# Chunk rows loaded in four pieces from ScalarE, and two VectorE steps moved, in a fused attention, MLP and soft-expert kernel

## The chip, the cores and the metric

The kernel runs on one core of one Trainium2 chip. The metric is the device time of one execution in microseconds, lower is better. Three runs of the kernel before took 622.63, 623.71 and 618.45 us (median 622.63). Device time is a little longer than the span of the profile, which goes from the first to the last instruction.

## The reference

Three stages in a row, all in float32. The first is a recurrence over 768 steps for each of 4 x 8 heads of width 48; the other two are an MLP of width 2048 on 3072 tokens of width 384, and soft experts with 32 slots.

```python
for t in range(S):                                   # attention, S = 768
    kt, vt, rt, wt = (k[:, :, t], v[:, :, t], r[:, :, t], w[:, :, t])
    cur = np.einsum('bhd,bhe->bhde', u[None] * kt, vt)
    y[:, :, t] = np.einsum('bhd,bhde->bhe', rt, state + cur)
    state = wt[:, :, :, None] * state + np.einsum('bhd,bhe->bhde', kt, vt)
...
h = x @ w_in                                         # MLP, x = y as 3072 x 384
x = (h * (1.0 / (1.0 + np.exp(-1.702 * h)))) @ w_out
...
logits = x @ phi                                     # soft experts
d = softmax(logits, over tokens);  c = softmax(logits, over slots)
slot_out = relu((d.T @ x) @ w1[e]) @ w2[e]           # for each expert's slots
out = c @ slot_out
```

## The kernel before

**Tiling.** The sequence of each batch is cut in 6 chunks of 128 steps, 24 chunks in all. For each chunk the four arrays w, r, k, v lie in one tile `raw[n % 2]` of 112 partitions (two heads of 48, with a gap) by 4 fields by 4 head pairs by 129 numbers, 903 KB; there are two such tiles. VectorE makes from it the running products of the decays (`decays`, a scan), their inverses (`invert`, a scan), r times decay (`decayed`), k times inverse (`grown_keys`), the bonus products r*u*k (`bonus`), and v times their sum over a head (`bonus_values`, tile `ybuf`). TensorE turns the keys (`turn_keys`), sums the bonus products, and in `meet(o, n)` does the scores and state sums of chunk n together with the outputs of chunk o. Then VectorE adds the outputs to `ybuf`, SyncE stores them to a scratch array and loads them back as columns x of the MLP.

**The MLP.** The chunks are grouped in 9 steps of 2, 2, 2, 3, 3, 3, 3, 3, 3 chunks (256 or 384 columns). Each step has 16 blocks (`NF`), one for every 128 of the 2048 hidden units, so there are 144 blocks, numbered F. In block F TensorE does the first layer of F (9 matmuls: `hps`, line 1377) and the second layer of F - 2 (6 or 9 matmuls: `acc`, line 1512). ScalarE does the activation `g` (line 845) and its rounded part `gh` (line 856), VectorE the rest `gl` (line 1149). Matmuls use split values (a high and a low part), so each product is three matmuls.

**Order.** There is no scheduler. A table written by hand, `part_at`, says in which block F each step of each chunk is issued (`place_parts`), and `meeting_at` says in which block the meetings lie. Within a block each engine goes through its own list of `if` statements in the order written. With f = 16 i the first block of step i, the meetings lie in blocks f + 3, f + 7 and f + 11, and the `bonus` steps one block ahead of each, in f + 2, f + 6 and f + 10.

**Who waits for whom.** The eighth bank of PSUM, `mps`, is used in turn by many steps; `mps_read` is what TensorE waits for before it writes there again. After the bonus sums it is `uv_done`, which `bonus_values` counts (line 1017). So a meeting waits on TensorE until `bonus_values` of the block before is done. `uv_done` is also what SyncE waits for before it loads a chunk's rows (`load_raw`, line 633) into the tile that the chunk two before has left. SyncE's queue holds, one after the other, those loads, the stores of `ybuf` (line 645), the loads of `vn` (line 640) and those of x (line 649). `rest_x` (line 539) makes the low part `xl` of x, which TensorE waits for at the start of a step.

Of the kernel before, what the change touches and what calls it, by code (L numbers as in the profile page):

```python
# [59 lines left out]
def attention_mlp_soft_experts(nc, dmaj, vnat, wall, ucol, w_in, w_out, phi, w1, w2, scratch, out):  # L60
# [8 lines left out]
    with ctx:  # L69
# [144 lines left out]
        decays_first = sem("decays_first")  # L214
        raw_in = [sem(f"raw_in{i}") for i in range(2)]
        vn_in = [sem(f"vn_in{i}") for i in range(2)]
        u_in = sem("u_in")
# [143 lines left out]
        place_parts(5, scan=17, invert=18, grow=18, turn=20, decayed=19, bonus_a=19, bonus_b=19, split=20, bonus=21)  # L361
        place_parts(6, scan=21, invert=22, grow=22, turn=24, decayed=24, bonus_a=23, bonus_b=23, split=24, bonus=25)
        meeting_at = {5: (None, 2), 9: (2, 3), 10: (3, None), 18: (None, 4), 22: (4, 5), 26: (5, 6)}
        for i in range(2, NST - 1):
            n, f = BASE[i + 1] + 1, NF * i
            place_parts(n, scan=f - 6, invert=f - 5, grow=f - 5, bonus_a=f - 3, bonus_b=f - 2, decayed=f - 1,
                        turn=f, split=f, bonus=f + 2)
            place_parts(n + 1, scan=f + 1, invert=f + 2, grow=f + 3, bonus_a=f + 4, bonus_b=f + 4, decayed=f + 5,
                        turn=f + 5, split=f + 5, bonus=f + 6)
            meeting_at[f + 3], meeting_at[f + 7], meeting_at[f + 11] = (n - 1, n), (n, n + 1), (n + 1, None)  # L370
            if i + 1 < NST - 1:
                place_parts(n + 2, scan=f + 6, invert=f + 7, grow=f + 7, bonus_a=f + 8, bonus_b=f + 8, decayed=f + 9,
                            turn=f + 9, split=f + 9, bonus=f + 10)
                meeting_at[f + 11] = (n + 1, n + 2)
# [256 lines left out]
        def _(sp):  # L631
# [43 lines left out]
            for n in range(NCH):  # L675
                if n <= FULL:
                    sp.wait_ge(uv_done, n + 1)
                    load_raw(n + 2)
                if FULL <= n < NCH - 3:
                    sp.wait_ge(uv_done, n + 2)  # L680
                    load_raw(n + 3)
                sp.wait_ge(y_done, n + 1)
# [87 lines left out]
        def _(act):  # L770
# [17 lines left out]
            def excesses(j):  # L788
# [48 lines left out]
            for F, gather, job in slots_of_work:  # L837
# [29 lines left out]
                if job == "exps":  # L867
                    exp_slots(act, 0)
                elif job not in (None, "shares"):
                    if job == 0:  # L870
                        act.wait_ge(y_stored[1], 32 * (NCH // 2 - 1))
                    high_slots(act, job)
                if (F, "split") in part_at:
                    n = part_at[F, "split"]
# [58 lines left out]
        def _(dve):  # L933
# [8 lines left out]
            def field(n, q):  # L942

                return raw[n % 2][:, q, :, 1:C + 1]

            def decays(n):

                if n == 0:
                    dve.wait_ge(decays_first, 16)
                else:  # L950
                    dve.wait_ge(raw_in[n % 2], 16 * (n // 2 + 1))
                flat = [t.rearrange("d p t -> d (p t)") for t in (decay[n % 2][:, :, :], raw[n % 2][:, W], restart[:, :, :])]
                dve.tensor_tensor_scan(flat[0], flat[1], flat[2], 1.0, ALU.mult, ALU.max).then_inc(scanned, 1)  # L953

            def bonus(n, half):

                if n == FULL and half == 0:
                    dve.wait_ge(u_in, 16)
                dve.wait_ge(raw_in[n % 2], 16 * (n // 2 + 1))
                for p in (2 * half, 2 * half + 1):  # L960
# [18 lines left out]
            def decayed(n):  # L979

                if n == 0:
                    dve.wait_ge(raw_in[0], 16)
                if n >= 2 * PRE:
# [6 lines left out]
            def grown_keys(n):  # L990

                dve.wait_ge(inverted, n + 1)
                dve.tensor_tensor(out=kd[n % 2][:, :, :], in0=field(n, KK), in1=inv[:, :, 1:C + 1], op=ALU.mult).then_inc(front, 1)

# [15 lines left out]
            def bonus_values(n):  # L1010

                dve.wait_ge(u_done, n + 1)
                if n >= 2 * PRE:
                    dve.wait_ge(y_stored[n % 2], 32 * (n // 2 - 1))
# [128 lines left out]
            for F, gather, job in slots_of_work:  # L1143
                if F is not None and F < NF * NST:
                    wide = SIZES[F // NF] * C
                    dve.wait_ge(gh_done, F + 1)
                    if F >= 2:
                        dve.wait_ge(mlp_done, F - 1)
                    dve.tensor_tensor(out=gl[F % 2][:, 0:wide], in0=g32[F % 2][:, 0:wide], in1=gh[F % 2][:, 0:wide].bitcast(fp32),  # L1149
                                      op=ALU.subtract).then_inc(gl_done, 1)  # L1150
                if (F, "scan") in part_at:
                    decays(part_at[F, "scan"])
                if (F, "invert") in part_at:
                    invert(part_at[F, "invert"])
# [18 lines left out]
                if F in low_at:  # L1173
                    low_part(low_at[F])
                if (F, "bonus") in part_at:
                    bonus_values(part_at[F, "bonus"])
                if F in meeting_at:
# [3 lines left out]
                    if n is not None:  # L1181
                        first_state(n)
                        mask_scores(n)
                        next_state(n)
                if F is not None and F < NF * NST and split_now(F):
# [552 lines left out]
```

## Time and profile before

| | us |
|---|---|
| median of 3 runs | 622.63 |
| lowest and highest | 618.45, 623.71 |
| the profiled execution | 620.75 |
| its span | 619.0 |

| Engine | busy us | share of the span |
|---|---|---|
| TensorE matmuls (PE) | 579.4 | 94% |
| TensorE weight loads (PEld) | 529.1 | 85% |
| VectorE (DVE) | 329.7 | 53% |
| ScalarE (ACT) | 261.0 | 42% |
| GpSimd (POOL) | 10.4 | 2% |

The mean granted clock of TensorE over the span is 0.984 of full speed. The DMA engines move 77.5 MB, 125 GB/s on average. A matmul in the profile overlaps the next, so its mean duration (340 ns) is longer than the distance between two (about 170 ns). "issue" as the releaser of a wait means that the profile shows nothing that the engine waited for. Issuing a DMA is not counted as busy time of the engine that does it.

### The profile page before, as it was taken

The numbers are of one execution on the slowest core, as the hardware profiler recorded it, in microseconds if no ns is written. First come the engines' busy times: TensorE is split into PE (matmuls) and PEld (weight loads), VectorE is DVE, ScalarE is ACT, GpSimd is POOL, SyncE is SP. The second block draws the span as 40 slices with busy tenths as digits, with TensorE's granted clock in tenths as the row PEclk, the third lists the DMA queues.
The fourth block names the chain that finished last, engine by engine and source line by source line (L and its number), as shares of the span: only waits on it lengthen the run. The fifth ranks groups of instructions, "written<-read, shape, count | busy, mean of one in ns | idle before, by whom it ended". The sixth has DMA issues, their size and how long they took to land.

```text
span 619.0 us, 15142 instructions
## 1 busy us (share of the span) xinstructions
PE 579.4 (94%) x6335; PEld 529.1 (85%) x6335; DVE 329.7 (53%) x713; ACT 261.0 (42%) x540; POOL 10.4 (2%) x28
## 2 busy tenths in 40 slices
PE   8989899799799999998999999997999999999993
PEld 6888888789689998998999999997999999998432
DVE  8688766557565664555545663665344323323314
ACT  4864443263343335333453335332533356554313
POOL 4010000000000000000000000000000000000000
PEclk9999999899899999999999999998999999999998
DMA  8995524304232331033303330333001089668637
GB/s 300 364 247 147 154 61 105 95 2 134 65 100 70 92 95 43 28 83 89 101 1 99 100 100 2 100 99 99 1 3 40 26 296 338 207 204 268 225 121 305
DMA packets 45301, 77.50 MB, mean 125 GB/s; under 512 B 3296, under 2 KB 32480, under 8 KB 42656
## 3 DMA queue, kind: packets, MB, share of 16 engines
q1 hardware_dynamic: 44432, 73.37, 38.2%
q0 software_dynamic: 800, 3.15, 1.5%
q8 instruction: 51, 0.84, 0.6%
q14 instruction: 18, 0.15, 0.1%
HBM read 67.46 MB, written 9.04 MB: 124 GB/s over the span
## 4 chain that ended last, share of the span: by engine, by line
PE 79%; DMA 9%; issue 5%; DVE 3%; ACT 2%; SPq 2%; ACTq 0%; DVEq 0%
PE hps L1377 31%; PE acc L1512 30%; DMA spare<-w_in 3%; DMA w2s<-w 2%; PE mps L1318 2%; DMA y_scratch<-ybuf 2%; PE zps L1300 2%; PE mps L1411 1%; PE mps L1595 1%; PE zps L1312 1%; PE mps L1628 1%; PE yps L1312 1%; DMA out<-obuf 1%; PE mps L1608 1%; PE hps L1672 1%
## 5 line engine op out<-in xcount | busy, mean ns | idle before, releaser
L1149 DVE TENSOR_TENSOR gl<-g,gh 128x384 fp32r<-128x384 f32 (+1 forms) x144 | 73.8, 513 | 228.5 <-ACT gh L856 228.3
L1377 PE MATMUL hps<-xh,wi_hi 128*128 128x384 f32 (+1 forms) x432 | 147.7, 342 | 3.7 <-DVE xl L539 2.0
L1377 PE MATMUL hps<-xh,wi_lo 128*128 128x384 f32 (+1 forms) x432 | 138.3, 320 | 9.3 <-issue 9.3
L1377 PE MATMUL hps<-xl,wi_hi 128*128 128x384 f32 (+1 forms) x432 | 137.9, 319 | 0.0
L845 ACT ACTIVATE g<-hps 128x384 f32<-128x384 f32 (+1 forms) x144 | 65.5, 455 | 168.0 <-PE hps L1377 167.7
L1512 PE MATMUL acc<-wo_hi,gh 128*128 128x384 f32 x384 | 130.3, 339 | 1.1 <-issue 1.1
L1512 PE MATMUL acc<-wo_hi,gl 128*128 128x384 f32 x384 | 130.6, 340 | 0.0
L1512 PE MATMUL acc<-wo_lo,gh 128*128 128x384 f32 x384 | 130.6, 340 | 0.0
L856 ACT ACTIVATE gh<-g 128x384 fp32r<-128x384 f32 (+1 forms) x144 | 70.5, 489 | 122.8 <-PE acc L1512 122.2
L1377 PEld LDWEIGHTS hps<-xh,wi_hi 128*128 128x128 f32 x432 | 82.1, 190 | 17.3 <-issue 8.9
L1377 PEld LDWEIGHTS hps<-xh,wi_lo 128*128 128x128 f32 x432 | 82.0, 190 | 3.5 <-issue 3.5
L1377 PEld LDWEIGHTS hps<-xl,wi_hi 128*128 128x128 f32 x432 | 82.3, 191 | 0.9
L1512 PEld LDWEIGHTS acc<-wo_hi,gh 128*128 128x128 f32 x384 | 73.2, 191 | 2.8 <-issue 2.7
L1512 PEld LDWEIGHTS acc<-wo_lo,gh 128*128 128x128 f32 x384 | 73.2, 191 | 1.3 <-issue 1.2
L1512 PEld LDWEIGHTS acc<-wo_hi,gl 128*128 128x128 f32 x384 | 73.2, 191 | 0.0
L977 DVE TENSOR_TENSOR_SCAN inv<-raw,ends 112x516 f32<-112x516 f32 x24 | 29.6, 1233 | 0.8
L953 DVE TENSOR_TENSOR_SCAN decay<-raw,restart 112x516 f32<-112x516 f32 x24 | 29.4, 1225 | 0.1
L1318 PE MATMUL mps<-vn,kn 64*48 64x48 f32 x640 | 24.0, 206 | 4.1 <-issue 4.0
L1318 PEld LDWEIGHTS mps<-vn,kn 64*48 64x48 f32 x640 | 20.6, 121 | 4.5 <-issue 4.1
L961 DVE SCALAR_TENSOR_TENSOR ruk<-raw,ucols 112x128 f32<-112x128 f32 x80 | 23.2, 345 | 0.0
L1312 PE MATMUL zps<-rp,state 48*48 48x64 f32 x320 | 21.8, 216 | 0.0
L1300 PEld LDWEIGHTS zps<-rp,kd 48*64 48x64 f32 x352 | 12.5, 134 | 9.8 <-issue 9.8
(251 smaller groups left out, 742.8 us busy)
## 6 DMA issues: line engine op xcount, KB each, us to landing
raw<-dmaj SPq DMA_DIRECT2D x23, 903.0 KB, 5.6
w1s<-w SPq DMA_DIRECT2D x16, 768.0 KB, 6.5
w2s<-w SPq DMA_DIRECT2D x16, 768.0 KB, 6.9
vn<-vnat SPq DMA_DIRECT2D x24, 192.0 KB, 3.2
tests<-wall SPq DMA_DIRECT2D x6, 768.0 KB, 14.9
out<-obuf SPq DMA_DIRECT2D x12, 384.0 KB, 3.9
y_scratch<-ybuf SPq DMA_DIRECT2D x44, 96.0 KB, 2.2
x<-y_scratch SPq DMA_DIRECT2D x22, 192.0 KB, 2.6
```

Of the source, the lines that this page charges most:

```text
L845: act.activation(g32[F % 2][:, 0:wide], hps[F % 2][:, 0:wide], ACT.Gelu_apprx_sigmoid).then_inc(gelu_done, 1)
L856: act.activation(gh[F % 2][:, 0:wide], g32[F % 2][:, 0:wide], ACT.Copy).then_inc(gh_done, 1)
L953: dve.tensor_tensor_scan(flat[0], flat[1], flat[2], 1.0, ALU.mult, ALU.max).then_inc(scanned, 1)
L961: last = dve.scalar_tensor_tensor(ruk[n % 2][:, p, :], field(n, RR)[:, p], ucols[:, p:p + 1], field(n, KK)[:, p], ALU.mult, ALU.mult)
L977: dve.tensor_tensor_scan(flat[0][:, ::-1], later, flat[1][:, ::-1], 1.0, ALU.mult, ALU.add).then_inc(inverted, 1)
L1149: dve.tensor_tensor(out=gl[F % 2][:, 0:wide], in0=g32[F % 2][:, 0:wide], in1=gh[F % 2][:, 0:wide].bitcast(fp32), op=ALU.subtract).then_inc ...
L1300: return pe.matmul(score_banks(n)[par][cols, p * HALF:(p + 1) * HALF], kd[n % 2][rows, p, cols], rp[n % 2][rows, p, cols], start=p == 0, s ...
L1312: return pe.matmul((zps, yps)[c][rows, p * HALF:(p + 1) * HALF], (state[o % 2], midway)[c][rows, p, :], rp[o % 2][rows, p, HALF * c:HALF * ...
L1318: return pe.matmul(sum_banks(n)[c][HALF * par:HALF * par + D, p * D:(p + 1) * D], kn[n % 2][rows, p, HALF * par:HALF * par + D], vn[n % 2] ...
L1377: last = pe.matmul(hps[F % 2][:, 0:wide], w[:, g, at:at + 128], v[i % 2][:, g, 0:wide], start=m == 0, stop=m == 3 * G - 1)
L1411: last = pe.transpose(mps[:, p * R:(p + 1) * R], kd[n % 2][:, p, :], ident[0:R, 0:R])
L1512: last = pe.matmul(acc[m][:, 0:DM], a[k][:, rows], w[:, f % CW, :], start=f == 0 and w is hi and a is gh, stop=f == NF - 1 and a is gl)
```

## The change

Three parts.

1. From chunk 4 on, a chunk's rows are no longer loaded by one DMA of 903 KB from SyncE, but by four of 226 KB from ScalarE, one for each field, in four different blocks given by `load_w`, `load_k`, `load_r`, `load_v` in the table. Each waits for the last reader of its field two chunks before, and each has its own semaphore (`field_in`), for which VectorE waits ahead of each use of the field. Bytes and destinations are the same. Chunks 0 to 3 are loaded as before. SyncE's waits for `uv_done` at those places go with the loads.
2. On VectorE, `bonus_values` stands directly behind `gl` of its block, ahead of the scans and the other steps of that block.
3. For chunk 2 (`PRE`), the mask of the scores and the next state are made in block 7, behind the keys of chunk 3, instead of in block 5.

```diff
+        field_in = [[sem(f"{name}_in{i}") for i in range(2)] for name in ("w", "r", "k", "v")]
...
+        place_parts(PRE, mask=7)
+        place_parts(4, load_w=7, load_k=8, load_r=9, load_v=10)
+        place_parts(5, load_w=15, load_k=16, load_r=17, load_v=18)
+        place_parts(6, load_w=19, load_k=20, load_r=21, load_v=23)
...
             place_parts(n, scan=f - 6, invert=f - 5, grow=f - 5, bonus_a=f - 3, bonus_b=f - 2, decayed=f - 1,
-                        turn=f, split=f, bonus=f + 2)
+                        turn=f, split=f, bonus=f + 2, load_w=f - 8, load_k=f - 7, load_r=f - 6, load_v=f - 4)
             place_parts(n + 1, scan=f + 1, invert=f + 2, grow=f + 3, bonus_a=f + 4, bonus_b=f + 4, decayed=f + 5,
-                        turn=f + 5, split=f + 5, bonus=f + 6)
+                        turn=f + 5, split=f + 5, bonus=f + 6, load_w=f - 2, load_k=f - 1, load_r=f, load_v=f + 1)
...
                 place_parts(n + 2, scan=f + 6, invert=f + 7, grow=f + 7, bonus_a=f + 8, bonus_b=f + 8, decayed=f + 9,
-                            turn=f + 9, split=f + 9, bonus=f + 10)
+                            turn=f + 9, split=f + 9, bonus=f + 10, load_w=f + 2, load_k=f + 4, load_r=f + 5, load_v=f + 6)
...
             for n in range(NCH):
-                if n <= FULL:
+                if n < PRE:
                     sp.wait_ge(uv_done, n + 1)
                     load_raw(n + 2)
-                if FULL <= n < NCH - 3:
-                    sp.wait_ge(uv_done, n + 2)
-                    load_raw(n + 3)
                 sp.wait_ge(y_done, n + 1)
...
+            def load_field(n, q):
+
+                wide = HP * (C + 1)
+                part = slice(q * wide + (q == RR), (q + 1) * wide + (q == W))
+                dst, src = (t.rearrange("d q p t -> d (q p t)") for t in (raw[n % 2], dmaj[n]))
+                act.dma_start(dst[:, part], src[:, part]).then_inc(field_in[q][n % 2], 16)
...
+                if (F, "load_v") in part_at:
+                    n = part_at[F, "load_v"]
+                    act.wait_ge(uv_done, n - 1)
+                    load_field(n, VV)
...
+                if (F, "bonus") in part_at:
+                    bonus_values(part_at[F, "bonus"])
                 if (F, "scan") in part_at:
                     decays(part_at[F, "scan"])
...
                 if (F, "grow") in part_at:
                     grown_keys(part_at[F, "grow"])
+                if (F, "mask") in part_at:
+                    mask_scores(part_at[F, "mask"])
+                    next_state(part_at[F, "mask"])
...
-                if (F, "bonus") in part_at:
-                    bonus_values(part_at[F, "bonus"])
```

What the diff doesn't tell is where the rows land on each engine. VectorE in block 17, where chunk 4's `bonus_values` (`ybuf<-mps,raw`, whose end TensorE's meeting in block 18 waits for) and chunk 5's first scan (`decay<-raw,restart`) both lie. Before:

```order
L1149 TENSOR_TENSOR gl_115<-g_1_110,gh_112 128x256
L953 SCALAR_TENSOR_TENSOR decay_71<-raw_67,restart 112x516
L1017 TENSOR_TENSOR ybuf_87<-mps,raw_68 112x512
L1149 TENSOR_TENSOR gl_114<-g_0_109,gh_111 128x256
L973 RECIPROCAL ends<-decay_71 112x4
L977 SCALAR_TENSOR_TENSOR inv<-raw_67,ends 112x516
```

The same place in the changed kernel:

```order
L1185 TENSOR_TENSOR gl_115<-g_1_110,gh_112 128x256
L1053 TENSOR_TENSOR ybuf_87<-mps,raw_68 112x512
L987 SCALAR_TENSOR_TENSOR decay_71<-raw_67,restart 112x516
L1185 TENSOR_TENSOR gl_114<-g_0_109,gh_111 128x256
L1008 RECIPROCAL ends<-decay_71 112x4
L1012 SCALAR_TENSOR_TENSOR inv<-raw_67,ends 112x516
```

The scan now stands behind `ybuf`. In the blocks f + 2 it is `RECIPROCAL` and the scan `inv` that stood ahead of `ybuf` and now stand behind it.

SyncE's queue around chunks 2 and 3, where the store of chunk 3's outputs (`y_scratch<-ybuf_87`) stands behind a load of rows. Before:

```order
L649 DMA x<-y_scratch 128x3x128
L633 DMA raw_68<-dmaj 112x2064 [waits uv_done]
L645 DMA y_scratch<-ybuf_87 48x4x128 [waits y_done]
L645 DMA y_scratch<-ybuf_87 48x4x128
L649 ISA [waits y_stored1]
```

The same place in the changed kernel:

```order
L654 DMA x<-y_scratch 128x3x128
L650 DMA y_scratch<-ybuf_87 48x4x128 [waits y_done]
L650 DMA y_scratch<-ybuf_87 48x4x128
L654 ISA [waits y_stored1]
```

The load is gone from this queue, and with it its wait. ScalarE in blocks 15 to 18, where the four loads of chunk 5 now lie (in the kernel before there was no DMA among these rows):

```order
L865 ACTIVATE gh_112<-g_1_110 128x256 [waits mlp_done,gelu_done]
L802 DMA raw_68<-dmaj 112x517 [waits inverted]
L854 ACTIVATE g_0_109<-hps 128x256 [waits gl_done,h_done]
L865 ACTIVATE gh_111<-g_0_109 128x256 [waits mlp_done,gelu_done]
L802 DMA raw_68<-dmaj 112x516 [waits ruk_made,front]
L904 ACTIVATE rukh<-ruk_79 112x512 [waits u_done,ruk_made]
L811 ACTIVATE kn_83<-mps 128x448 [waits meetings,kd_turned]
L854 ACTIVATE g_1_110<-hps 128x256 [waits gl_done,h_done]
L861 ACTIVATE x_116<-acc 128x384 [waits mlp_done]
L861 ACTIVATE x_116<-acc 128x384
L865 ACTIVATE gh_112<-g_1_110 128x256 [waits mlp_done,gelu_done]
L802 DMA raw_68<-dmaj 112x515 [waits ruk_made,decayed_done]
```

Each load stands directly behind `gh` of its block, ahead of the block's other steps. TensorE's instructions are the same ones in the same order.

## Rows read from the trace of the kernel before

**Rows 1.** The page's first lines, and the queue that fetches instructions: packets, MB, share.
```profile
span 619.0 us, 15142 instructions
PE 579.4 (94%) x6335; PEld 529.1 (85%) x6335; DVE 329.7 (53%) x713; ACT 261.0 (42%) x540; POOL 10.4 (2%) x28
...
q8 instruction: 51, 0.84, 0.6%
```

**Rows 2.** Waits of the matmuls, all that matter here: us in total, times, longest.
```profile
PE hps L1377 <- issue: 9.3, 3, 3.4
PE mps L1318 <- issue: 4.0, 1, 4.0
PE zps L1300 <- DVE ybuf L1017: 2.7, 4, 0.9
PE hps L1377 <- DVE xl L539: 2.0, 1, 2.0
...
PE mps L1411 <- DVE kd L993: 1.1, 1, 1.1
...
PE zps L1300 <- issue: 1.1, 1, 1.1
PE acc L1512 <- issue: 1.1, 1, 1.1
```

**Rows 3.** Windows, four idle stretches: length, busy us of each engine, PEclk, DMA share, GB/s.
```profile
109.96:113.92 3.96, 0.05 (x2) 0.05 (x4) 0.07 (x1) 0.00 (x0) 0.00 (x0) 1.00 0.32 90
155.58:158.89 3.31, 0.05 (x1) 0.06 (x1) 1.50 (x5) 0.00 (x0) 0.00 (x0) 1.00 0.51 115
281.38:283.96 2.58, 0.06 (x1) 0.06 (x1) 1.52 (x5) 0.00 (x0) 0.00 (x0) 1.00 0.38 83
426.52:429.94 3.42, 0.05 (x1) 0.04 (x1) 2.58 (x8) 0.00 (x0) 0.00 (x0) 0.82 0.46 116
```

**Rows 4.** Timeline of SyncE's queue: start, duration; three of five loads of rows.
```profile
106.91 0.33 SPq L633 DMA_DIRECT2D raw<-dmaj  x1
...
276.74 0.33 SPq L633 DMA_DIRECT2D raw<-dmaj  x1
...
422.94 0.33 SPq L633 DMA_DIRECT2D raw<-dmaj  x1
```

**Rows 5.** DMA view of 419 to 427.3 us: busy tenths in 40 slices, then the queues.
```profile
DMA  0000000000000000000000092093798999595967
...
q1 hardware_dynamic: 118, 0.92, 39.1%
```

**Rows 6.** DMA view of the next 1.7 us, 427.3 to 429.
```profile
q8 instruction: 1, 0.02, 4.8%
```

**Rows 7.** Windows at half clock, and one of the same length behind the first.
```profile
114.76:118.18 3.42, 3.42 (x15) 3.42 (x15) 2.48 (x8) 0.38 (x1) 0.00 (x0) 0.51 0.38 85
118.18:121.60 3.42, 3.42 (x27) 3.42 (x26) 2.71 (x5) 1.34 (x4) 0.00 (x0) 1.00 0.29 93
...
429.94:435.62 5.68, 5.68 (x20) 5.58 (x20) 0.00 (x0) 0.84 (x2) 0.00 (x0) 0.50 0.27 76
```

**Rows 8.** Timeline of VectorE in block 17.
```profile
81.66 1.23 DVE L953 TENSOR_TENSOR_SCAN decay<-raw,restart 112x516 f32<-112x516 f32 x1
82.80 0.67 DVE L1017 TENSOR_TENSOR ybuf<-mps,raw 112x512 f32<-112x512 f32 x1
```

**Rows 9.** The chain that ended last: start, us; chunk 3's store.
```profile
65.62 5.75 DMA y_scratch<-ybuf
```

**Rows 10.** Timeline of VectorE where step 1 of the MLP begins.
```profile
74.60 0.56 DVE L539 TENSOR_TENSOR xl<-x,xh 128x384 fp32r<-128x384 f32 x1 [0.92 <-ACT xh L447]
```

**Rows 11.** The page's last part: count, KB, median us to landing.
```profile
y_scratch<-ybuf SPq DMA_DIRECT2D x44, 96.0 KB, 2.2
...
raw<-dmaj SPq DMA_DIRECT2D x1, 226.2 KB, 2.7
```

**Rows 12.** A group of ScalarE: busy us, mean ns, idle us before it and releaser.
```profile
L856 ACT ACTIVATE gh<-g 128x384 fp32r<-128x384 f32 (+1 forms) x144 | 70.5, 489 | 122.8 <-PE acc L1512 122.2
```

More of the change, by code:

```diff
@@ L872, in _ @@
                     high_slots(act, job)
+                if (F, "load_w") in part_at:
+                    n = part_at[F, "load_w"]
+                    act.wait_ge(inverted, n - 1)
+                    load_field(n, W)
+                if (F, "load_k") in part_at:
+                    n = part_at[F, "load_k"]
+                    act.wait_ge(front, n - 1)
+                    act.wait_ge(ruk_made, n - 1)
+                    load_field(n, KK)
+                if (F, "load_r") in part_at:
+                    n = part_at[F, "load_r"]
+                    act.wait_ge(decayed_done, n - 1)
+                    act.wait_ge(ruk_made, n - 1)
+                    load_field(n, RR)
+                if (F, "load_v") in part_at:
+                    n = part_at[F, "load_v"]
+                    act.wait_ge(uv_done, n - 1)
+                    load_field(n, VV)
                 if (F, "split") in part_at:
@@ L944, in field, with await_field @@
                 return raw[n % 2][:, q, :, 1:C + 1]
+            def await_field(n, q):
+                if n < FULL:
+                    dve.wait_ge(raw_in[n % 2], 16 * (n // 2 + 1))
+                else:
+                    dve.wait_ge(field_in[q][n % 2], 16 * (n // 2 - FULL // 2 + 1))
             def decays(n):
@@ L950, in decays @@
                 else:
-                    dve.wait_ge(raw_in[n % 2], 16 * (n // 2 + 1))
+                    await_field(n, W)
                 flat = [t.rearrange("d p t -> d (p t)") for t in (decay[n % 2][:, :, :], raw[n % 2][:, W], restart[:, :, :])]
@@ L958, in bonus @@
                     dve.wait_ge(u_in, 16)
-                dve.wait_ge(raw_in[n % 2], 16 * (n // 2 + 1))
+                await_field(n, RR)
+                await_field(n, KK)
                 for p in (2 * half, 2 * half + 1):
@@ L979, in decayed @@
             def decayed(n):
-                if n == 0:
-                    dve.wait_ge(raw_in[0], 16)
+                await_field(n, RR)
                 if n >= 2 * PRE:
@@ L992, in grown_keys @@
                 dve.wait_ge(inverted, n + 1)
+                await_field(n, KK)
                 dve.tensor_tensor(out=kd[n % 2][:, :, :], in0=field(n, KK), in1=inv[:, :, 1:C + 1], op=ALU.mult).then_inc(front, 1)
@@ L1012, in bonus_values @@
                 dve.wait_ge(u_done, n + 1)
+                await_field(n, VV)
                 if n >= 2 * PRE:
@@ L1182, in _ @@
                         first_state(n)
-                        mask_scores(n)
-                        next_state(n)
+                        if n != PRE:
+                            mask_scores(n)
+                            next_state(n)
                 if F is not None and F < NF * NST and split_now(F):
```

## The prediction

> **What bounds the kernel now.** I read the page's head first: matmuls are busy 94% of the span [rows 1], and between about 100 and 560 us the blocks of the MLP follow each other on TensorE without a gap that VectorE or ScalarE causes, save a few. TensorE's own work is not touched by the change. So the question is only which idle stretches of TensorE go, and which come.
>
> The waits of the matmuls [rows 2] give the list. In the MLP region four lines carry it. First, 14.4 us in five stretches with the releaser "issue": 9.3 us in three before `hps`, 4.0 before `mps`, 1.1 before `acc`. Second, 2.7 us in four stretches before a meeting, for `ybuf` of line 1017, and one more stretch of 1.1 us before a meeting (`zps`, "issue"). Third, 2.0 us for `xl` when step 1 begins. Fourth, 1.1 us for `kd`.
>
> The first item is the large one, and its name tells nothing. The windows show the four longest: they begin at 109.96, 155.58, 281.38 and 426.52 us [rows 3], and in them TensorE has nothing to do. SyncE's queue [rows 4] issued a load of a chunk's rows at 106.91, 276.74 and 422.94 us, 3.05, 4.64 and 3.58 us ahead of such a stretch; for the second and for the fifth (1.1 us, in step 3) it is the same, so all five follow a load. The DMA view says what lies between. From 419 to 427.3 us it lists the hardware queue alone, 118 packets, and the engines are full from the load's first packet to the end of that window [rows 5]; no instruction packet. In the next 1.7 us there is one, on q8 [rows 6]. That queue brought 0.84 MB in 51 packets, 16 KB each, and TensorE has 12,670 matmuls and weight loads, about 250 for each packet [rows 1]. My reading: TensorE ran out of instructions, because the block that it had asked for stood behind 903 KB of rows. A meeting, with its many small matmuls back to back, uses them up fastest. And the load falls just there because one event, `uv_done`, starts both the load and the meeting.
>
> The idleness costs twice. Behind the first and the last of the four stretches the granted clock is at its lower level, 1.2 of 2.4 GHz: 3.42 us with 15 matmuls, against 27 in the 3.42 us behind it, and 5.68 us at 0.50 while TensorE is busy throughout [rows 7]; behind the second it is 3.42 us again. The three idle stretches that it follows are those of 3.31, 3.42 and 3.96 us; behind the one of 2.58 us [rows 3] it does not fall.
>
> **The change part by part.**
>
> *Loads in four.* Removed: 20 loads of 903 KB from SyncE. Added: 80 of 226 KB from ScalarE, the same bytes. Three things come of it.
>
> (a) No load is issued by `uv_done` any more. The pieces before a meeting (blocks f + 2, f + 6, f + 10) are issued behind `gh` of their block, about a block ahead of the meeting, and each should keep the DMA engines busy for a quarter of the 3.5 us or so that the whole one fills in [rows 5] (17 of 40 slices of 8.3 us), 0.9 us. The fetch should then start at once. What it needs after that is bounded by rows: at the last long stretch its packet starts after 427.3 and TensorE is back at 429.94, so at most 2.6 us. The time from the old load's issue to the end of the instructions was 3.05, 3.58 and 4.64 us. With 2.6 us nothing is left; if the fetch takes 1 us to start, 3.6 us, the first keeps 0.5 us; with 2 us, 1.5 and 1.0 us. I take 1.0 us left of 14.35 (3.96 + 3.31 + 2.58 + 3.42 + 1.08): **-13.35 us**. Bounds: 14.35 if nothing is left, 8 if pieces, stores and `vn` loads still delay some.
>
> (b) With no stretch of 3.3 us the clock has no reason to fall. At half clock half of the work's time is lost: (3.42 + 3.42 + 5.68) / 2 = **-6.25 us**. Bounds: 6.25, and 0 to 3 if one or two long ones stay.
>
> (c) SyncE's queue is relieved. Chunk 3's store took 5.75 us to land [rows 9], right behind the load of chunk 5, where 2.2 is the median [rows 11]. Up to 3.5 us come off, and x lands that much earlier. But VectorE was idle only 0.92 us for `xh` before `xl` [rows 10]; before that it was in the scan of chunk 4. So of TensorE's 2.0 us, 0.92 go: **-0.95 us** with rounding. Bounds 0 (a piece of chunk 4 beside chunk 2's store) and 2.0. Later steps have x long before.
>
> What it costs: 80 issues at 0.33 us [rows 4] are 27 us on ScalarE, and four waits per chunk. ScalarE sat idle 122.8 us just before `gh` [rows 12] (0.85 us in a block); the issue stands behind `gh`, so `gl` isn't behind it, and what it takes comes out of the wait before the next `gh`. Taken at nothing; should that cover fail, a block loses what an issue exceeds 0.85 us by. The waits name steps at least 3 blocks back, so they find their counts reached. VectorE's new waits: every piece has 2 blocks or more until its first use, 5 to 7 us, and 226 KB landed in 2.7 us at the start of the kernel among others [rows 11]. Nothing.
>
> *Bonus behind `gl`.* In block 17 the scan takes 1.23 us ahead of `ybuf` [rows 8], and TensorE sits idle from 82.66 us until it ends. In the other four stretches a scan stands ahead in the same way. The scans are longer than each of the waits (0.9 at most, and 1.10), so all of 2.7 + 1.1 = **-3.80 us** goes. The sums it reads are done before `gl` is, since TensorE does them right behind the matmuls that `gh` waits for. The scan comes 0.6 us later, with a block to spare. Bounds 2.5 and 3.8. In the blocks of 384 columns nobody waited, but the earlier `uv_done` lets TensorE's queue run on sooner, which is on the side of (a).
>
> *Mask of chunk 2.* About 1 us of VectorE goes from block 5 to block 7. Ahead of `kd` of chunk 3, `gl` of block 7 waits for `gh` anyway, so `kd` comes when it came and the wait of 1.1 us stays; behind it, `decayed` and the products of chunk 3 come 1 us later, still ahead of their meeting. 0; bounds -1.1 and +1.0.
>
> **Sum:** 619.0 - 13.35 - 6.25 - 0.95 - 3.80 = 594.65 us of span. Around it lie 1.75 us (620.75 - 619.0), so 596.4. The profiled execution is 1.9 us under the median of the three; I say **597**.
>
> **A rule that speaks against it.** The Trainium skill, "DMA: Bandwidth & Descriptors", Rules for kernel authors, wants transfers of 1 MiB or more, and says that spreading them over the issuing engines doesn't help bandwidth. By it the change is a step back. No row here makes bandwidth the limit, since the rows are moved a block or more before their use; by the rule the sum would be the same.
>
> **Rivals.**
>
> *The stalls have another cause.* The load and the end of the instructions would both follow from `uv_done`, without one holding up the other. Then stalls and clock stay, and only (c) and the bonus count: 620.75 - 4.75 = 616. For it: one queue's packets needn't stop another's. Against it: in 419 to 427.3 us no instruction packet moved though TensorE ran dry at 426.52, and one came as the load ended [rows 5, 6]. The Trainium skill, "DMA: Bandwidth & Descriptors", Queues, rings and completion order, says that each engine takes turns between queues packet by packet, and "Runtime: NRT & Kernel Launch", Instruction fetch mechanics, that fetches of 16 KiB are mostly hidden; by these this rival is the right one. The size agrees with the 0.84 MB in 51 packets; hidden they were not, by the rows above. Chance 0.11.
>
> *Part of it stays.* One or two long stretches remain, with their fall of the clock, because a piece meets a store and a `vn` load at a fetch: 3.4 + 2.8 us each, so 603 to 609. Chance 0.14.
>
> *More collisions, slower.* A piece has as many rows as the whole had, only shorter ones. If what holds a fetch up is the number of rows queued and not their bytes, a piece blocks as long as a load did, and there are 80 instead of 20. Five of 20 loads hit before. Say the five stay and as many come anew, at (14.35 + 6.25) = 20.6 us for five: 620.75 - 4.75 + 20.6 = 637. It decides from a hold of 3 us for a piece. Against it: 226 KB landed in 2.7 us, issue and all, where 903 KB take twice that. Chance 0.05.
>
> *Forecast*, 592 to 602: chance 0.70.
>
> **Range.** Around 597: all gains at their upper bounds give 594.4 (14.35, 6.25, 3.8 and 2.0 off 620.75), and the executions before scatter by some 2 us around it, so 592. Upwards I go over the case of stalls that stay in part, to 610; outside lie 616, 637 and a little below 592. A measurement of this kernel tells 1%, 6 us, from no change. Faster by more (under 616.4): the forecast, the part case, and half of the first rival, 0.89. Within 1%: the other half, 0.06. Slower: 0.05.
>
> **What would show it.** Right: no wait for "issue" of over 1.5 us among the matmuls between 100 and 560 us; granted clock 1.00 there; no wait of a meeting for `ybuf`; chunk 3's store lands in about 3 us; ScalarE's idle time before `gh` shrinks by less than the 27 us of issues and no line of matmuls waits for `g` or `gl` anew. Wrong: "issue" waits at the same places (then the load was not the cause), instruction packets that still start late beside a piece, DMA issues on ScalarE of over 1 us, or VectorE waiting for `raw`.

## The result: 3.9% faster, and the profile after

Four runs of the changed kernel gave a median of 597.6 us (595.2 to 598.4), beside 622.2 us (618.5 to 623.7) for the kernel before on the same chip. The ratio is 0.961, with a 95% interval from 0.955 to 0.966. The profiled execution took 598.3 us, with a span of 596.6. The forecast was 597. Medians here and below are of all runs on record; the ratios leave out two slow ones, one of experiment 5 and one of the kernel before beside experiments 9 to 11.

The head of the page and the queues come first. TensorE is busy for 96% of the span [rows 1], and `q10` is ScalarE's queue, which is new: 10,240 packets, 128 for each of 80 pieces.

```profile
span 596.6 us, 15329 instructions
PE 573.4 (96%) x6335; PEld 523.4 (88%) x6335; DVE 329.6 (55%) x713; ACT 264.0 (44%) x540; POOL 10.5 (2%) x28
...
q10 hardware_dynamic: 10240, 18.50, 10.1%
```

The waits of the matmuls follow (total, times, longest). Of the seven lines of [rows 2] four are left, each smaller. The 14.35 us for "issue" in five stretches are now 0.9 before `mps`, at an old place, and 0.2 before `acc`, at 61.1 us, where none was before. All of `zps` for `ybuf` or "issue" is gone, `xl` is half, and a wait of a meeting for `rp` is new.

```profile
PE hps L1417 <- DVE xl L544: 1.0, 1, 1.0
PE mps L1358 <- issue: 0.9, 1, 0.9
...
PE zps L1340 <- DVE rp L1021: 0.5, 1, 0.5
PE mps L1451 <- DVE kd L1028: 0.5, 1, 0.5
...
PE acc L1552 <- issue: 0.2, 1, 0.2
```

Windows of the same kernel say what became of the longest stretch and of the clock (length, busy us of each engine, clock, DMA share, GB/s). The first row is where a stretch of 3.96 us was [rows 3]; the second lies where 15 matmuls in 3.42 us ran at half clock [rows 7], and has 54 in twice that time. The third is the whole region: granted clock 1.00.

```profile
109.26:110.16 0.90, 0.05 (x2) 0.05 (x4) 0.07 (x1) 0.00 (x0) 0.00 (x0) 1.00 0.06 21
...
114.00:120.83 6.83, 6.83 (x54) 6.07 (x53) 3.82 (x11) 4.35 (x10) 0.00 (x0) 1.00 0.27 87
...
40.00:560.00 520.00, 515.83 (x5695) 483.27 (x5697) 288.53 (x631) 230.02 (x487) 3.17 (x4) 1.00 0.35 109
```

The DMA view of 107.3 to 110.2 us has a piece and an instruction packet, ahead of the stretch of 0.90 us. The piece was issued at 107.39 us. The instruction packet starts at 107.45 (the first busy tenths of the view) and the piece's own packets only at 108.3, so this fetch didn't stand behind that piece; experiment 10 has most of this stretch without any load.

```profile
DMA  0090000000000093735799899511100000000000
...
q10 hardware_dynamic: 128, 0.23, 25.8%
q8 instruction: 1, 0.02, 2.6%
```

**The bill.** I added up every idle stretch of TensorE over 0.2 us from 40 us on to the end of the MLP: 21.3 us before, 3.6 after, so 17.7 us less. With half of the 12.5 us at half clock, 6.25, that is 23.9. The spans differ by 22.4. Of the rest 1.1 us is the start: the matmul that waits there for `g` began at 33.57 us before and at 34.64 after, ahead of the first piece at 51.06. That wait comes out at 1.4 to 2.2 us in the kernels of this study with or without pieces (all but experiment 7's, 0.5), so I count it as scatter.

### The profile page after: what moved, and what is told of

Its sections match the earlier page's. It is cut to its first block, busy times and chain, and to the rows that moved or that the text cites. A ratio compares the mean times of both kernels' runs of the same rounds, so it can differ in the third digit from the quotient of the medians.

```text
span 596.6 us, 15329 instructions
## 1 busy us (share of the span) xinstructions
PE 573.4 (96%) x6335; PEld 523.4 (88%) x6335; DVE 329.6 (55%) x713; ACT 264.0 (44%) x540; POOL 10.5 (2%) x28
## 3 DMA queue, kind: packets, MB, share of 16 engines
q10 hardware_dynamic: 10240, 18.50, 10.1%
## 4 chain that ended last, share of the span: by engine, by line
PE 83%; DMA 7%; DVE 3%; issue 3%; ACT 2%; SPq 2%; ACTq 0%; DVEq 0%
PE hps L1417 33%; PE acc L1552 32%; DMA spare<-w_in 4%; DMA w2s<-w 2%; PE zps L1340 2%; PE mps L1358 2%; PE yps L1352 1%; PE mps L1451 1%; PE mps L1635 1%; PE zps L1352 1%; PE mps L1668 1%; PE zps L1346 1%; DMA out<-obuf 1%; PE mps L1648 1%; PE hps L1712 1%
## 5 line engine op out<-in xcount | busy, mean ns | idle before, releaser
L854 ACT ACTIVATE g<-hps 128x384 f32<-128x384 f32 (+1 forms) x144 | 65.6, 455 | 146.4 <-PE hps L1417 146.2
L1552 PE MATMUL acc<-wo_hi,gl 128*128 128x384 f32 x384 | 129.2, 337 | 0.0
L1552 PE MATMUL acc<-wo_lo,gh 128*128 128x384 f32 x384 | 129.2, 336 | 0.0
L1552 PE MATMUL acc<-wo_hi,gh 128*128 128x384 f32 x384 | 129.0, 336 | 0.2 <-issue 0.2
L865 ACT ACTIVATE gh<-g 128x384 fp32r<-128x384 f32 (+1 forms) x144 | 70.5, 489 | 118.1 <-PE acc L1552 117.5
L1352 PE MATMUL yps<-rp,midway 48*48 48x64 f32 x320 | 20.7, 216 | 0.0
```

Of the source, the lines that this page charges most:

```text
L854: act.activation(g32[F % 2][:, 0:wide], hps[F % 2][:, 0:wide], ACT.Gelu_apprx_sigmoid).then_inc(gelu_done, 1)
L865: act.activation(gh[F % 2][:, 0:wide], g32[F % 2][:, 0:wide], ACT.Copy).then_inc(gh_done, 1)
L1352: return pe.matmul((zps, yps)[c][rows, p * HALF:(p + 1) * HALF], (state[o % 2], midway)[c][rows, p, :], rp[o % 2][rows, p, HALF * c:HALF * ...
L1552: last = pe.matmul(acc[m][:, 0:DM], a[k][:, rows], w[:, f % CW, :], start=f == 0 and w is hi and a is gh, stop=f == NF - 1 and a is gl)
```

## The experiments

Each is told with its edit, what was expected, and what came. Medians are those of the kernel and of the kernel before on the same chip.

**1. The two reorderings alone.** The kernel before, with the bonus products behind `gl` and the mask moved; the loads stay whole, on SyncE.

```diff
+        place_parts(PRE, mask=7)
...
                                       op=ALU.subtract).then_inc(gl_done, 1)
+                if (F, "bonus") in part_at:
+                    bonus_values(part_at[F, "bonus"])
                 if (F, "scan") in part_at:
```

> The kernel before with only the VectorE order of the change (bonus_values directly behind gl, chunk 2's mask behind chunk 3's keys); rows still loaded by SyncE at uv_done in one piece. Theory (the load holds back TensorE's instruction fetch): the 3.8 us of waits for ybuf go; and where a scan stood ahead of bonus_values, uv_done and so the load come 1.15 us earlier against the fetch, so the idle stretches of 3.31, 1.08, 2.58 and 3.42 us shrink to about 2.7, 0, 1.4 and 2.3, while that of 3.96 us in block 26, where nothing stood ahead, stays; the clock falls once instead of three times. Together 12 us: about 608.5. Rival (the parts simply add, the stalls do not depend on when the load comes): only 3.8 us, 617.

Measured: 616.5 against 624.0, ratio 0.988 (0.983 to 0.992). The waits for `ybuf` are gone, as are 3.0 us of the stalls: TensorE is idle for "issue" in the same five places, for 4.25, 2.74, 1.12, 1.15 and 2.12 us. Those that shrank are three of meetings where a scan used to stand ahead (3.31, 2.58 and 3.42 before). But the clock fell more often. The windows, first an idle stretch and then what follows it:

```profile
74.09:76.11 2.02, 0.05 (x1) 0.05 (x1) 0.98 (x2) 1.19 (x3) 0.00 (x0) 0.98 0.42 141
...
76.07:79.48 3.41, 3.41 (x14) 3.41 (x15) 1.63 (x3) 0.44 (x2) 0.00 (x0) 0.51 0.00 0
...
425.18:427.30 2.12, 0.04 (x1) 0.04 (x1) 2.09 (x7) 0.00 (x0) 0.00 (x0) 1.00 0.06 16
...
113.61:120.44 6.83, 5.36 (x33) 5.27 (x34) 2.77 (x8) 0.63 (x2) 0.00 (x0) 0.50 0.26 60
157.99:164.81 6.82, 6.26 (x25) 6.17 (x26) 1.47 (x5) 1.67 (x4) 0.00 (x0) 0.50 0.32 75
427.64:431.05 3.41, 3.41 (x12) 3.41 (x11) 0.16 (x1) 0.49 (x1) 0.00 (x0) 0.51 0.54 148
```

TensorE is busy for 18.4 us at half clock, so 9.2 us are lost to it, 3.0 more than before. Then -3.8 (`ybuf`) -3.0 (stalls) +3.0 (clock) is -3.8, and the spans differ by 3.7. What the reordering saved in stalls went into the clock. So the 608.5 us that I expected did not come: the stall of 1.08 us did not go, and the clock fell four times instead of once. The time is the rival's 617, but not for the rival's reason, since three stalls did shrink. It also ended my remark that the clock follows stretches of 3.3 us or more: here it is low behind 2.02 us at `xl`, where before it stayed up behind 2.0 at the same place.

**2. The loads alone.** The changed kernel with bonus and mask back in their old places (the edit of experiment 1 taken out again).

```diff
-        place_parts(PRE, mask=7)
...
-                if (F, "bonus") in part_at:
-                    bonus_values(part_at[F, "bonus"])
                 if (F, "scan") in part_at:
```

> The changed kernel with bonus_values and chunk 2's mask back at their old places; only the four loads from ScalarE are new. Theory: stalls for issue and the falls of the clock are gone as in the changed kernel, the waits of the meetings for ybuf (3.8 us) are back: about 601.5. Rival (the order of VectorE is what took the stalls away): 615 or more, with stalls of over 2 us for issue.

Measured: 602.1 against 624.0, ratio 0.966 (0.963 to 0.970), clock 0.992. All stalls over 1 us are gone from `hps`, `mps` and `acc` without the new order, and the waits of the meetings are back:

```profile
PE zps L1335 <- DVE ybuf L1052: 2.8, 4, 0.9
...
PE zps L1335 <- issue: 1.1, 1, 1.1
...
PE hps L1412 <- issue: 0.9, 2, 0.6
PE mps L1353 <- issue: 0.9, 1, 0.9
```

So the loads bring most of the gain, 21.9 us here, and the order adds the 3.9 us of the first two lines; by profiled spans it is 600.7 - 596.6 = 4.1.

**3. Whole loads, elsewhere.** The changed kernel, but ScalarE issues one load of 903 KB in a block away from the meetings.

```diff
-                        turn=f, split=f, bonus=f + 2, load_w=f - 8, load_k=f - 7, load_r=f - 6, load_v=f - 4)
+                        turn=f, split=f, bonus=f + 2, load=f - 8)
...
+                if (F, "load") in part_at:
+                    n = part_at[F, "load"]
                     act.wait_ge(uv_done, n - 1)
+                    act.dma_start(raw[n % 2][:, :, :, :], dmaj[n]).then_inc(raw_in[n % 2], 16)
```

> The changed kernel, but a chunk's rows in one load of 903 KB from ScalarE, in blocks f + 4, f + 8 and f + 14 instead of four loads: none of these is the block ahead of a meeting. Theory (what counts is that no load stands ahead of the fetch that a meeting needs): as fast as the changed kernel, 597 to 600, fetches start up to 4.4 us late but at places with more than 7 us in hand. Rival (what counts is the size of a load): stalls of 2 to 4 us come back, at other places, 605 to 620.

Measured: 600.5 against 624.0, ratio 0.961 (0.958 to 0.965), which the changed kernel's 0.961 (0.955 to 0.966) can't be told from. It is half a us over the range expected. One stall of note is left:

```profile
PE acc L1535 <- issue: 1.6, 1, 1.6
```

It stands at 62.2 us, behind the load of chunk 4, issued at 55.03 us; the fetch's packet starts at 61.38. This load was put in block 8, and in the first steps the meetings lie in blocks 5, 9, 10, 18, 22 and 26, so it is the one load that does stand directly ahead of a meeting. In the same 8 us (53 to 61.3) the engines also moved 0.79 MB of GpSimd's weight loads. It is enough, then, to move the load away from the meeting; it need not be cut. Nor does the issuing engine matter for what a fetch meets: behind ScalarE's whole loads issued at 104.67 and 123.41 us a packet starts 4.46 and 4.41 us later, as behind SyncE's, and TensorE is idle for it for 0.1 us at most.

**4. Pieces, at the old moment.** The kernel before, with SyncE issuing four DMAs back to back where it issued one.

```diff
             def load_raw(n):
...
+                    for q in range(4):
+                        part = slice(q * wide, (q + 1) * wide)
+                        sp.dma_start(dst[:, part], src[:, part]).then_inc(raw_in[n % 2], 16)
```

> The kernel before, but from chunk 4 on the rows are loaded by four DMAs issued one right behind the other by SyncE at the old moment, uv_done. Theory (a fetch waits for all bytes queued ahead of it): the same 903 KB stand ahead of the fetch, the five stalls stay within half a us, 618 to 623. Rival (a fetch can slip in between two DMAs): it waits for a quarter, the stalls are gone and the time is near 601.

Measured: 605.3 against 624.0, ratio 0.973 (0.969 to 0.977), clock 0.993. My theory, that a fetch waits for all bytes that were queued ahead of it, fell. The same bytes are asked for in the same moment, and the stalls shrink to 0.98, 0.26 and 0.59 us. SyncE's timeline and the DMA view of 410.2 to 412.3 us show how: the four issues begin at 410.24, and the fetch's packet is there before 412.3, while the last pieces still come (the four land 2.7, 3.6, 4.5 and 5.6 us after the first issue).

```profile
410.24 1.75 SPq L640 DMA_DIRECT2D raw<-dmaj  x4
```
```profile
q1 hardware_dynamic: 150, 0.28, 47.7%
q8 instruction: 1, 0.02, 3.2%
```

In the kernel before, no instruction packet came in 4.36 us from the issue at 422.94 [rows 4, 5]. The packets' start times say the same of the other stalls: the fetch starts 3.4 to 4.6 us after the issue of a whole load, and 1.8 to 2.5 after the first of four pieces. At the loads where nobody waits it starts 1.8 to 4.4 us after the first piece, mostly 3 and more. One reading is that a fetch waits for what the load's queue held when the DMA engine turned to it, and not for what is added behind; when a fetch was asked for isn't in the traces, so this is not shown. What is shown is that cutting alone takes most of the stalls away, and that is 2.7%.

**5. Halves at the old moment.** As 4, but two DMAs of 451 KB.

```diff
+                    for q in range(2):
+                        part = slice(q * wide, (q + 1) * wide)
+                        sp.dma_start(dst[:, part], src[:, part]).then_inc(raw_in[n % 2], 16)
```

> The kernel before, but from chunk 4 on a chunk's rows in two DMAs of 451 KB one right behind the other by SyncE at uv_done. With four of 226 KB the fetches started about 2 us after the first piece was issued instead of 4.4, and the stalls were 0, 1.0, 0.3, 0 and 0.6 us. Theory after that (a fetch waits for the DMA under way on its engine, not for those queued behind it): half the data under way, a start about 2.5 to 3 us after the first issue, stalls of about 2, 1.7, 0, 1, 1.7 us, at most one or two falls of the clock: 606 to 612. Rival (the fetch waits for all bytes, and the four pieces were fast for another reason): 618 or more.

Measured: 617.0 against 623.5, ratio 0.988 (0.983 to 0.992), clock 0.981: between whole and quarters, and nearer to the whole. Its two long stretches:

```profile
154.94:158.25 3.31, 0.04 (x1) 0.05 (x1) 1.51 (x5) 0.00 (x0) 0.00 (x0) 0.89 0.56 129
424.88:426.93 2.05, 0.06 (x1) 0.05 (x1) 2.02 (x7) 0.00 (x0) 0.00 (x0) 1.00 0.53 140
```

The fetches at these two start 4.5 and 2.9 us after the first issue, the one as behind a whole load; at two more they start 3.5 and 2.4 us after it, with 1.08 and 0.39 us idle, and the longest stretch of before, 3.96 us, is gone. The wait for `xl` is 3.6 us instead of 2.0, with half clock behind it, which is a part of why halves gain so little. By the profiles, the stalls for "issue" are 6.8 us (3.31, 1.08, 0.39 and 2.05), close to the 6.4 that I had expected, so 7.5 less than before. But `xl` takes 1.6 us more, and TensorE is busy for some 16.4 us at half clock instead of 12.5, so 1.9 us more are lost: -7.5 + 1.6 + 1.9 = -4.0, and the spans differ by 4.1. Of that half clock 3.41 us come at 34.67 us, in the start, ahead of any half load. My range of 606 to 612 was missed by the clock and `xl`, not by the stalls.

**6 and 7. The program shifted.** The kernel before, with 20 (then 50) small matmuls more at its start. Each is a weight load and a matmul, so all that follows stands 40 (100) instructions later in TensorE's program.

```diff
+                keep_warm((32,) * 20)
                 pe.wait_ge(made, 10 + EG)
```

> The kernel before with 20 matmuls of 32 columns more at the head of TensorE's start-up (40 instructions with their weight loads, under 1 us of work). They move every later instruction by 40 places against the borders of the fetched blocks of 256, and change nothing else. Theory (the stalls are late instruction fetches): of the five stalls none stays where it was (blocks 26, 39, 59, 71, 107); counted on the trace of before, the borders then fall badly in about block 51 (near 2 us) and 99 (under 1 us) only, so stalls add up to 2 to 5 us instead of 14.4 and the clock falls at most once: 600 to 608, faster than before by some 15 us for more work. Rival (the load delays a step of the program, not its fetch): the stalls stay in their five places, 619 to 624.

Measured with 20: 628.7 against 623.5, ratio 1.013 (1.005 to 1.021). The stalls are in other operations than in [rows 2], where `hps` had 9.3 us and `mps` 4.0:

```profile
PE mps L1318 <- issue: 9.9, 3, 4.3
PE yps L1312 <- issue: 3.3, 1, 3.3
PE zps L1312 <- issue: 3.0, 1, 3.0
...
PE acc L1513 <- issue: 2.0, 1, 2.0
```

Counted in TensorE's instructions, the stretches keep to borders 256 apart, and are thus 40 instructions earlier in the work. Four of the five fall in the same meetings, one is gone, and two are new: 1.95 us at 204.54 and 1.49 us at 58.89 us. Of the 7.9 us by which the spans differ, 1.2 are the start, 3.8 the stalls (18.2 us in all), and 3.7 the clock: 19.9 us of TensorE's busy time are at half clock, against 12.5. The wait for `xl` is 1.0 us less. What I had expected of the stalls' number was wrong: I had them end where the border is passed well before the load is issued, and such a fetch was held as well.

> As the run with 20 matmuls more, but with 50, which is 100 instructions. Theory: counted on the trace of before, the borders fall badly near blocks 43 (3 us) and 75 (4 us) and slightly near 36, so two stalls long enough for a fall of the clock: 607 to 614. Rival: five stalls in the old places, 620 to 625.

Measured with 50: 629.5 against 623.5, ratio 1.013 (1.006 to 1.019), against 607 to 614 us expected. The spans differ by 7.0 us. Most of that is the start itself: the matmuls added are followed by 6.83 us at half clock, and the first `hps` of the MLP comes at 36.45 us instead of 29.50; the wait for `g` behind it gives 1.2 us of this back. The idle stretches for "issue" are 2.80, 0.51, 1.63, 2.84 and 3.43 us, 11.2 in all and 3.1 less than before, and four of the five are in other blocks. The clock takes that back: some 19.4 us at half clock against 12.5, so 3.4 us more are lost. Even without its start it is far above what I expected. Which loads hurt depends on how long the program ahead of them is; my rule for it failed twice, so how far ahead a fetch is asked for stays open.

**8. The changed kernel shifted.** The same 20 matmuls in the changed kernel.

```diff
+                keep_warm((32,) * 20)
                 pe.wait_ge(made, 10 + EG)
```

> The changed kernel with the same 20 matmuls more. Theory: with short loads away from the meetings the place of the borders no longer matters, 595 to 600 and no stall for issue over 1.2 us. Rival (the changed kernel is fast by a lucky place of its borders): stalls of 2 us and more appear, 603 to 612.

Measured: 599.8 against 623.5, ratio 0.965 (0.957 to 0.973), which overlaps the changed kernel's. The gain isn't luck of one alignment: between 100 and 560 us the longest stretch is 0.82 us, and the clock stays up. But my bound of 1.2 us for a stall did not hold. One of 1.9 us is left, at 59.67 us, in a meeting of the first steps, at the border where the shifted kernel before has one of 1.49 us and experiment 3 its 1.6:

```profile
PE mps L1358 <- issue: 2.7, 2, 1.9
```

The fetch's packet starts at 59.09 us. Between 53.4 and 59 us the DMA engines carried 0.68 MB of pieces and 0.72 MB of a weight load from GpSimd; which of them held it wasn't separated. So the pieces make the kernel insensitive to the borders in the region of the large stalls, and not everywhere.

**9. A large DMA put back.** The changed kernel, and SyncE issues a DMA of 786 KB to an unused place at the old moment of the load.

```diff
+                if FULL <= n < NCH - 3:
+                    sp.wait_ge(uv_done, n + 2)
...
+                    sp.dma_start(dst.rearrange("(p x) -> p x", p=128),
+                                 src.rearrange("(p x) -> p x", p=128)).then_inc(extra, 16)
```

> The changed kernel, and at the old moments (uv_done, chunks 4 to 20) SyncE issues a DMA of 786 KB of the same rows to an unused place of the scratch array, which nobody reads. Nothing waits for its data except the next such DMA. Theory (one large DMA under way at the start of a meeting holds back the fetch): stalls for issue of 2 to 4 us come back after meetings, three to five of them, with falls of the clock, 608 to 620. Rival (the old stalls came from the tile's reuse or from SyncE's order): 597 to 600, no stall over 1 us.

Measured: 607.1 against 625.6, ratio 0.972 (0.968 to 0.977), against 0.961 (0.955 to 0.966) without it. The stalls return at their old places, the clock falls behind one of them:

```profile
PE hps L1426 <- issue: 5.1, 3, 2.5
```
```profile
148.26:150.77 2.51, 0.05 (x1) 0.05 (x1) 2.10 (x7) 0.00 (x0) 0.00 (x0) 1.00 0.30 74
414.20:416.28 2.08, 0.05 (x1) 0.04 (x1) 2.05 (x7) 0.00 (x0) 0.00 (x0) 1.00 0.05 12
152.22:155.64 3.42, 3.42 (x17) 3.32 (x16) 1.48 (x5) 1.28 (x3) 0.00 (x0) 0.51 0.46 125
```

Nothing waits for this DMA's data, so the cause is shown: a large transfer beside the fetch. The size is small: 6.5 us by profiled spans, of which the two stretches above and one of 0.53 us are 5.1 and the clock 1.7, and 607.1 us is just under the 608 to 620 that I expected. A stretch of 0.7 us at 60.3 us comes before the first of these DMAs, at 93.8 us, and is not theirs. The transfer is smaller than a load, and `uv_done` comes earlier by the new order, as the two stretches of 2.08 and 2.12 (experiment 1) at one place suggest; which of the two counts for more was not separated.

**10. No loads of chunks 4 to 23.** The changed kernel without its 80 pieces and the waits for them; the data of these chunks are wrong.

```diff
-                if (F, "load_w") in part_at:
-                    n = part_at[F, "load_w"]
-                    act.wait_ge(inverted, n - 1)
-                    load_field(n, W)
...
```

> The changed kernel without the loads of chunks 4 to 23 and without the waits for them (those chunks are computed from the rows of chunks 2 and 3, so the output is not the reference's). It shows what the 80 short loads still cost. Theory: nearly nothing, the stall of 0.9 us in block 26 goes, 595 to 597 where the changed kernel takes 597.6. Rival (they still hold TensorE or ScalarE up somewhere): below 594.

Measured: 596.0 against 625.6, ratio 0.953 (0.949 to 0.958). Against the changed kernel's own ratio of 0.961 the intervals just overlap: the 80 pieces with their 18.5 MB still cost 0.8% at the middle of the two, and 596.6 - 595.3 = 1.3 us by profiled spans. This profile has 3.4 us at half clock in the start, at 34 us, which the changed kernel's has not; without that loss of 1.7 us it would be some 3 us. Nor is the stretch at 109 us the pieces' alone: 0.60 us of its 0.90 are there without any load, where I had expected it to go.

**11. The mask back in block 5.** The changed kernel with chunk 2's mask where it was.

```diff
-        place_parts(PRE, mask=7)
...
-                        if n != PRE:
-                            mask_scores(n)
-                            next_state(n)
+                        mask_scores(n)
+                        next_state(n)
```

> The changed kernel with chunk 2's mask and next state back in block 5. Prediction's view: worth nothing, within 0.5 us of the changed kernel. Rival from the trace of after (the wait for kd fell from 1.1 to 0.5 us, and two short ones of 0.5 us came in blocks 8 and 9): the mask behind the keys moved 0.7 us from one wait to two others; taking it back gives one wait of 1.1 us again and removes the 0.5 us before the meeting of block 9, again within 0.5 us.

Measured: 597.0 against 625.6, ratio 0.955 (0.952 to 0.958), beside 0.961 (0.955 to 0.966): no difference that can be told. No version here clearly beats the changed kernel.

## Why the prediction was right

**Stalls, -13.35 us.** Measured: 14.35 became 1.1, so -13.2. The largest is 0.9 us, within the 1.5 us that the prediction set as its test, and experiments 3, 4 and 9 show the cause from both sides. That 1.0 us would be left was right in part by luck: I took it for a fetch that starts 1 to 2 us late beside a piece, but at the stretch of 0.9 us the packet starts ahead of the piece's, 2.65 us before TensorE's next matmul, and 0.60 us of it stay without any load (experiment 10). One step of the reasoning was too coarse. I wrote that the fetch stood behind 903 KB of rows. Experiment 4 queues the same bytes in the same moment, and the fetch starts in the middle of them. Nor did a packet come only "as the load ended" in the kernel before: behind the load issued at 422.94 us it starts after 4.38 us, the load's last large packets end after 5.29, and the load lands after 5.70.

The first rival leaned on the Trainium skill, "DMA: Bandwidth & Descriptors", Queues, rings and completion order: each DMA engine takes turns between queues packet by packet. I took a packet for something short. The section lets one hold some 9 to 17 descriptors. In the profile's count a whole load moves in packets of about 8 KB (118 packets, 0.92 MB [rows 5]), so about 7 on each of 16 engines, which could be one turn. Read so, the rule doesn't contradict the traces; how much one turn takes was not measured, so no run here shows that it is what held the fetch. The page's section Rules for kernel authors, with its 1 MiB or more for a transfer, speaks of bandwidth, and there was no lack of that; what smaller transfers gave here, 2.7% without any move (experiment 4), is not weighed by it.

**Clock, -6.25 us.** Exact for the region: 1.00 from 40 to 560 us. The condition that I gave for it, no stretch of 3.3 us or more, was wrong: experiment 1 has the lower clock behind 2.02 us, experiment 7 behind 1.63. The term survived because the longest stretch left in that region is 0.97 us (`xl`), not because of where I had put the limit; in that the term was lucky. Where the stalls only shrank, in experiment 1, the clock took back what they gave.

**Meetings, -3.80 us.** None of their waits at `zps` for `ybuf` or "issue" is left, and experiment 2 has 3.9 us of them again.

**`xl`, -0.95 us.** 2.0 became 1.0 us. Chunk 3's store, two halves at 66.0 us, lands in 2.9 us at most, where it was 5.75 [rows 9]:

```profile
L650 SPq DMA_DIRECT2D y_scratch<-ybuf x2: 443/469/495, 66.0 to 66.6; - x2
...
DMA to landing us min/median/max: 2.3/2.4/2.9
```

The rest is VectorE in the inverse scan at 74.27 us, as argued: x has long been there.

**ScalarE's 27 us of issues, nothing.** They are in neither wait that matters. Its idle time before `gh` fell from 122.8 us [rows 12] to 118.1, and that before `g` from 168.0 to 146.4:

```profile
L854 ACT ACTIVATE g<-hps 128x384 f32<-128x384 f32 (+1 forms) x144 | 65.6, 455 | 146.4 <-PE hps L1417 146.2
...
L865 ACT ACTIVATE gh<-g 128x384 fp32r<-128x384 f32 (+1 forms) x144 | 70.5, 489 | 118.1 <-PE acc L1552 117.5
```

The 26.3 us together are the issues. They came out of the wait for `g`, not of that for `gh` as I had said, since an issue ends before the next `hps` does.

**The waits on ScalarE, nothing.** Here I was wrong, by 0.5 us, and one of my signs of being wrong did show: one of the 80 issues took over 1 us. I said that they name steps at least three blocks back. The first does not: the piece in block 7 waits for chunk 3's inverse, which VectorE makes in block 7. The two timelines, ScalarE first:

```profile
51.06 2.25 ACTq L802 DMA_DIRECT2D raw<-dmaj  x1
53.36 1.49 ACT L782 ACTIVATE wo_hi<-stage 128x1536 fp32r<-128x1536 f32 x1 [2.21 <-DVE inv L1012]
```
```profile
51.73 1.23 DVE L1012 TENSOR_TENSOR_SCAN inv<-raw,ends 112x516 f32<-112x516 f32 x1
...
55.60 0.42 DVE L1185 TENSOR_TENSOR gl<-g,gh 128x256 fp32r<-128x256 f32 x1 [0.98 <-ACT gh L865]
55.94 0.68 DVE L1021 TENSOR_TENSOR rp<-raw,decay 112x512 f32<-112x512 f32 x1
```

The issue is held until the scan ends at 52.96, `wo_hi` comes 2.2 us late, `gh`, `gl` and `rp` behind it, and TensorE waits 0.47 us for `rp` at 56.56. That wait, of 0.4 to 0.6 us, is in every kernel with pieces from ScalarE (experiments 2, 8, 9 and 11 too) and not in experiments 1, 3, 4 and 10.

**Mask, 0.** Experiment 11 agrees. The wait for `kd`, 1.1 us, did change: it is 0.37 and 0.46 now. That is the new place of the bonus products, since the split is there in experiment 11 without the mask's move, and experiment 2 has 1.13 us whole.

**Rivals.** The first, another cause, is excluded by experiment 9. Its number, 616, is what the order alone gave (experiment 1), by another sum. "Part of it stays", 603 to 609, did not come in this kernel, but did in 4 and 9. Of collisions anew, at 637, there is little: no new stretch of over 0.2 us for "issue" in the changed kernel, and one of 1.9 us when it is shifted (experiment 8).

## What to carry over

An idle stretch of TensorE that is put down to "issue" deserves a look at the instruction queue: if its packet comes only 3 to 5 us after a large load was issued, the load should be cut into pieces or moved away from the stage that uses up instructions fastest. Here the cut alone gave 2.7%, and whole loads elsewhere, with the new order, 3.9%. Shorten such stretches to 1 us or less and not halfway, since the clock fell behind 1.6 and 2 us as behind 4. An unrelated edit that shifts the program can move these stalls, so a kernel that has them should be compared with a shifted copy of itself before a small gain or loss is believed.

## What the runs showed of the hardware

- From the start of the fetch's packet to TensorE's next matmul it took 2.2 to 2.9 us at every idle stretch of 0.5 us and more for a late fetch (2.5 to 2.7 in the kernel before, 2.4 to 2.9 in experiment 1, 2.2 to 2.7 in experiment 9).
- In the kernel before, an instruction packet starts 3.4 to 5.0 us after the issue of each of the loads of 903 KB from 83 us on, at the five where TensorE ran dry (3.4 to 4.6) and at those where it didn't. So a late fetch was the rule; that TensorE had enough instructions left at the others fits this, but isn't seen in a trace.
- The granted clock was low behind idle stretches of 2.02, 2.12, 2.74 and 4.25 us (experiment 1), and behind one of 1.63 us (experiment 7), and stayed high behind one of 2.58 us [rows 3] and one of 2.08 us (experiment 9). The length of the last stretch alone does not decide it; what else does was not tried.
